# Gram products of a chunked delta rule spread over eight steps in half fills, and k, q loads moved behind the q products

## The reference

```
k_n = k / (norm(k) + 1e-6)
for t in range(768):
    y[t]  = q[t] @ state
    v_old = state^T k_n[t]
    state = state + beta[t] * outer(k_n[t], v[t] - v_old)
```

## Time and profile before

| | us |
|---|---|
| median of 3 runs | 1146.16 (1144.45 to 1147.41) |
| the profiled execution | 1137.16 |
| its span | 1135.4 |
| PE busy in the span | 1029.8 (91%) |
| DVE busy | 869.6 (77%) |
| ACT busy | 779.8 (69%) |
| POOL busy | 227.7 (20%) |
| first copy_low of the recurrence starts at | 60.27 |
| last copy_low of the recurrence starts at | 293.76 |

### The profile page before, as it was taken

How to read it: one execution, slowest core, us unless ns; L and a number is a source line. 1 busy time by engine, 2 the same in 40 slices (tenths; PEclk the granted TensorE clock), 3 DMA queues, 4 the chain that set the end, 5 groups by cost and what they waited for, 6 DMA issues and landing times.

```text
span 1135.4 us, 24237 instructions
## 1 busy us (share of the span) xinstructions
PE 1029.8 (91%) x10274; PEld 819.1 (72%) x10280; DVE 869.6 (77%) x948; ACT 779.8 (69%) x991; POOL 227.7 (20%) x380
## 2 busy tenths in 40 slices
PE   4478788898778999999999998899999999999997
PEld 2366566666657788777787776778888888888886
DVE  4965646565389888788887877999787878888885
ACT  1143524465488998999998897987676767676764
POOL 5088887780010001001001000000000000000000
PEclk7588979899889999999999999999999999999999
DMA  7823434232343343524324353530100101010000
GB/s 176 238 59 103 114 99 128 73 88 98 101 91 77 74 112 63 123 55 112 74 55 111 74 147 89 136 111 1 56 1 10 45 0 56 0 56 1 29 1 28
DMA packets 35104, 86.99 MB, mean 77 GB/s; under 512 B 4416, under 2 KB 12096, under 8 KB 35008
## 3 DMA queue, kind: packets, MB, share of 16 engines
q1 hardware_dynamic: 27584, 59.13, 17.3%
q0 software_dynamic: 6912, 25.17, 11.6%
q10 hardware_dynamic: 512, 1.31, 0.5%
HBM read 46.27 MB, written 14.16 MB: 53 GB/s over the span
## 4 chain that ended last, share of the span: by engine, by line
PE 33%; DVE 20%; ACT 12%; issue 6%; DMA 1%; ACTq 0%; DVEq 0%; POOLq 0%
PE o_ps L854 6%; PE o_ps L856 6%; PE o_ps L855 6%; PE h_ps L854 5%; PE h_ps L856 5%; PE h_ps L855 5%; DVE val L1078 5%; DVE den L1035 5%; ACT rec L942 4%; DVE pa L1041 4%; ACT rec L950 3%; DVE val L1062 2%; ACT pa L918 2%; DMA val<-pa 1%; DVE den L1069 1%
## 5 line engine op out<-in xcount | busy, mean ns | idle before, releaser
L854 PE MATMUL o_ps<-g_hi,w_hi_early 128*128 128x512 f32 x288 | 115.5, 401 | 21.8 <-DVE g_lo L1084 15.7
L931 ACT ACTIVATE g_hi<-val 128x1024 fp32r<-128x1024 f32 x96 | 101.9, 1062 | 42.5 <-DVE val L1078 36.8
L845 POOL DMA_DIRECT2D val<-pa x48 | 41.5, 864 | 427.4 <-DVE pa L1041 427.4
L854 PE MATMUL o_ps<-g_hi,w_hi_late 128*128 128x512 f32 x288 | 114.4, 397 | 8.8 <-DVE g_lo L1084 8.3
L1062 DVE TENSOR_TENSOR val<-val,rec 128x1024 f32<-128x1024 f32 x96 | 117.0, 1219 | 5.6 <-DMA val<-pa 5.6
L1078 DVE SCALAR_TENSOR_TENSOR val<-den,val 128x1024 f32<-128x1024 f32 x96 | 117.4, 1223 | 5.0
L1084 DVE SCALAR_TENSOR_TENSOR g_lo<-val,g_hi 128x1024 fp32r<-128x1024 f32 x96 | 117.7, 1226 | 2.0 <-ACT g_hi L931 2.0
L855 PE MATMUL o_ps<-g_lo,w_hi_early 128*128 128x512 f32 x288 | 113.5, 394 | 0.0
L856 PE MATMUL o_ps<-g_hi,w_lo_early 128*128 128x512 f32 x288 | 113.3, 393 | 0.0
L855 PE MATMUL o_ps<-g_lo,w_hi_late 128*128 128x512 f32 x288 | 112.9, 392 | 0.0
L856 PE MATMUL o_ps<-g_hi,w_lo_late 128*128 128x512 f32 x288 | 112.8, 392 | 0.0
(11 more groups left out here) (114 smaller groups left out, 2179.7 us busy)
## 6 DMA issues: line engine op xcount, KB each, us to landing
val<-pa POOLq DMA_DIRECT2D x48, 512.0 KB, 4.6
w_raw<-w SPq DMA_DIRECT2D x16, 768.0 KB, 5.1
kv_run<-kv_n SPq DMA_DIRECT2D x24, 384.0 KB, 3.7
x_raw<-x_dram SPq DMA_DIRECT2D x12, 768.0 KB, 5.7
kq<-kq_t SPq DMA_DIRECT2D x44, 192.0 KB, 4.7
x_dram<-stage SPq DMA_DIRECT2D x12, 384.0 KB, 4.3
x_dram<-stage SPq DMA_DIRECT2D x6, 768.0 KB, 4.1
out<-stage SPq DMA_DIRECT2D x5, 768.0 KB, 4.1
```

The source lines that it names most:

```text
L854: nc.tensor.matmul(dst, hi, rhs_hi, start=first, stop=False)
L931: act_fn(g_hi[:, n % 2], val[:, n % 2], ACT.Copy, scale=-1.0).then_inc(g_hi_ready, 1)
```

## The change

The fills are cut in two halves by chunk (`c2` 0 or 1), and the halves are spread by written lists. In tiles 2 and 3 (and by the same rule wherever the tile exists) steps 0 to 3 do the second half of tile tau+2 and steps 4 to 7 the first half of tile tau+3, half a fill a step. Tiles 0 and 1 have lists of their own, with some whole fills, in which the order reaches the new shift. `scale_gram` follows the second half of a fill. `weights` of tile tau+3 moves to step 5 (step 7 in tile 0), and the transpositions of tile 2's n_mat to step 7 of tile 0. The wait ahead of `keep_warm` names the fills that are in flight then. On SP the kq loads go ahead of the kv load and wait for the q product of the chunk (`q_done`) instead of its update.

```diff
+GRAM_0 = ((), ((2, 0, 0), (2, 0, 1)), ((2, 1, 0),), ((2, 1, 1),), ((2, 2, 0), (2, 2, 1)), ((2, 3, 0),), ((2, 3, 1),),
+          ((3, 0, 0), (3, 0, 1)))
+GRAM_1 = (((3, 1, 0), (3, 1, 1)), ((3, 2, 0),), ((3, 2, 1),), ((3, 3, 0), (3, 3, 1)),
+          ((4, 0, 0),), ((4, 0, 1),), ((4, 1, 0),), ((4, 1, 1),))
+GRAM = ((2, 2, 0), (2, 2, 1), (2, 3, 0), (2, 3, 1), (3, 0, 0), (3, 0, 1), (3, 1, 0), (3, 1, 1))
...
+def gram_parts(tau, s):
+    if tau < 2:
+        return (GRAM_0, GRAM_1)[tau][s]
+    ahead, f, c2 = GRAM[s]
+    return ((tau + ahead, f, c2),) if tau + ahead < T else ()
...
                 for c in range(CT):
+                    if tau + RING < T:
+                        sp.wait_ge(q_done, index(tau, c, 1) + 1)
+                        for r in range(HALVES):
+                            load_kq(sp, tau + RING, c, r)
                     if tau + 1 < T:
                         sp.wait_ge(st_done, index(tau, c, 1) + 1)
                         load_kv(tau + 1, c)
-                    if tau + RING < T:
-                        for r in range(HALVES):
-                            load_kq(sp, tau + RING, c, r)
...
-            def gram_fill(j, f):
+            def gram_fill(j, f, chunks=range(2)):
                 cp, r = f // 2, f % 2
                 if r == 0:
-                    for c2 in range(2):
+                    for c2 in chunks:
                         pe.wait_ge(kq_loaded[slot(j, 2 * cp + c2)], 32 * (j // RING) + 32)
-                if j >= 2:
+                if j >= 2 and 0 in chunks:
                     pe.wait_ge(gram_used, 4 * j + f)
...
-                for c2 in range(2):
+                for c2 in chunks:
...
-                last.then_inc(gram_done, 1)
+                if 1 in chunks:
+                    last.then_inc(gram_done, 1)
...
                     if tau and s == 0:
                         pe.wait_ge(inv_ready, tau)
-                        if tau + 1 < T:
-                            pe.wait_ge(gram_used, 4 * (tau + 1) + 4)
+                        pe.wait_ge(gram_used, 4 * 3 + 1 if tau == 1 else min(4 * (tau + 2) + 2, 4 * T))
                         by_event()
                         keep_warm(BURST)
                     solve(tau, c, g)
-                    if tau + 2 < T and 0 <= fill < 4:
-                        gram_fill(tau + 2, fill)
+                    for j, f, c2 in gram_parts(tau, s):
+                        gram_fill(j, f, (c2,))
...
-                    if fill == 0 and tau + 2 < T:
-                        weights(tau + 2)
-                    if tau + 2 < T and 0 <= fill < 4:
-                        scale_gram(tau + 2, fill)
+                    if (tau, s) == (0, 1):
+                        weights(2)
+                    if (tau, s) == (0, 7):
+                        turn_n(2, 0, half_k)
+                        turn_n(2, half_k, C)
+                    if s == (7 if tau == 0 else 5) and tau + 3 < T:
+                        weights(tau + 3)
+                    for j, f, c2 in gram_parts(tau, s):
+                        if c2 == 1:
+                            scale_gram(j, f)
...
-                    if fill == 3 and tau + 2 < T:
+                    if tau and s == 3 and tau + 2 < T:
                         turn_n(tau + 2, 0, half_k)
-                    if fill == 4 and tau + 2 < T:
+                    if tau and s == 4 and tau + 2 < T:
                         turn_n(tau + 2, half_k, C)
```

More of the change, by code:

```diff
@@ L464, in _ @@
                     q = index(tau, c, g)
-                    fill = s - (1 if tau == 0 else 0)
                     if tau and s == 0:
                         pe.wait_ge(inv_ready, tau)
-                        if tau + 1 < T:
-                            pe.wait_ge(gram_used, 4 * (tau + 1) + 4)
+                        pe.wait_ge(gram_used, 4 * 3 + 1 if tau == 1 else min(4 * (tau + 2) + 2, 4 * T))
                         by_event()
```

## The result

The changed kernel is faster: median 1131.72 us over 6 runs (1131.49 to 1137.32) beside 1145.31 for the kernel before in the same job (6 runs, 1141.35 to 1147.41). The ratio is 0.9914, 95% interval 0.9891 to 0.9938, some 10 us. (The medians alone lie 13.6 us apart, because four of the changed kernel's six runs are near 1131.6 and the other two at 1135.0 and 1137.3.) I had forecast 4 us slower.

What follows compares the result with a forecast made beforehand. The recurrence was taken as bound by TensorE's own in-order stream. Terms 1.03 + 3.1 + 1.1 + 0.0 − 2.06 + 0.9 = +4.1 us, added to the timed median 1146.16, gave 1150.2 us; range 1142 to 1155.5.

Steps and rivals of the forecast that it cites:

- the one on the loads: kq issued about 2 us earlier, ahead of kv, in time for its use: cost 0, bad end 1 us in each of tiles 1 and 2.
- Rival A: Faster: parted load bursts shrink instruction-fetch stalls (−5.2 us) and clock falls (−2.2): 1142.8 us; chance 0.22.
- The sign that I had set for being wrong: One of three: the recurrence's "issue" idle, 20.8 us over three listed products, falling under 18 us.
- C: Slower still: idle in step 2 of tiles 1 and 2 and the border trip the low clock: 1155 us; chance 0.13.
- Bound by PE's in-order stream: Recurrence: steps run back to back on PE, about 0.3 us of cover each; a half fill costs 0.52 us, nearly all exposed.
- Tile 0, step 7: 4.1 us of DVE transpositions, weights and scaling before the state copy, against 0.90 idle: about 3.1 us on the path.
- Step 2 of tiles 1 and 2: Losing a half fill gains nothing; PE's idle time for u_blk grows from 1.75 to 2.27 us.
- Tile 3: Four half fills fewer and no squares to wait for: −2.06 us.
- Tiles 1 and 2: Half fills removed and added, less what is hidden: +1.1 us in tile 1, 0.0 in tile 2.
- The clock at the border of tiles 0 and 1: PE idles some 2.2 us before the warm-up, which may run at the low clock: 0 to 2.4 us, taken as 0.9.

Runs made afterwards that it cites:

- the loads alone: Kernel before with only the kq loads moved behind the q products, Gram fills left whole in steps 0 to 3: 0.9906 of before.
- before_shift128: Kernel before with 128 semaphore increments on PE's queue during its wait for the first inverse: 1.0046 of before.
- no_jam: Changed kernel, tile 0 keeping whole fills and transpositions in place, weights(3) in step 6, tile 3's first fill halved over steps 6 and 7: 0.9936 of before.

## Why the prediction was wrong

**The step that failed** is the one on the loads: "Cost 0, with 1 us in each of tiles 1 and 2 as the bad end." I asked only whether kq comes in time and what waits on SP. It does come in time. The term measured −0.73%, 8 us over three placements, from what the transfers do to an engine that never waits for them. With it the sum of +4.1 becomes −4, and the mean over placements is −4.3 us (0.9949 against 0.9987). The other 5 to 6 us of the measured 10 are the placement of this kernel, which no sum over a profile gives.

**The rival was there and I argued it away.** Rival A had the cause, the parted bursts and the fetches, and its 3.4 us under the kernel before is near the mean over placements, though not near the measured 10. Its mechanism was half right: it took most of its gain from less stall time in all (−5.2 us). The sum doesn't fall. It is 26.8 to 28.7 us in the six profiles of the kernel before and the loads alone, and 24 to 32 in all kernels but before_shift128; what changes with the loads is the length of single pieces and the time at the low clock. The sign that I had set for being wrong, stall time under 18 us, was met by the three lines that I had listed (14.3) and not by the whole (28.1): I had left out the k product and the Gram fills. A piece of 2.14 us was followed by 6.8 us at the low level in the earlier trace rows; that price I gave to the rivals A and C and not to the forecast, which left the 24 us at the low clock in tiles 1 and 2 as they were.

The Trainium skill (DMA: Bandwidth & Descriptors, "Queues, rings and completion order") has the DMA engines take turns between queue rows. I concluded that a fetch wouldn't stand behind a burst and let that weigh against A. The fetch packets agree with the page as far as they go: they take 1.1 us with and without load data beside them. My conclusion doesn't hold: 384 KB more per chunk cost 0.6% with nothing waiting for it, and fetches beside load data were followed by a long piece ten times as often.

**Bound by PE's in-order stream**: right. A half fill in a clean step pushes the q product back by 0.58 us, more than the 0.52 I took (half of the 1.03 in the earlier trace rows):

```profile
163.38 0.65 PE L374 MATMUL side_ps<-kq 48*32 48x64 f32 x32
163.96 0.54 PE L418 MATMUL y_bank<-state,kq 128*32 128x96 f32 x16
```

Spreading products gained nothing, as forecast: the half fills cost 0.36% on average, 4.1 us. That it is my sum to the decimal is luck, since the mean is only good to some 3 us and the sum's parts were off both ways.

**Tile 0, step 7**: right for the stretch itself. The residual to the state copy takes 3.96 us, where "4 us" stood, with the transpositions, the weights and the scaling between them; compare 0.90 of idle time in the earlier trace rows.

```profile
97.33 0.35 DVE L678 TENSOR_TENSOR z<-kv_run,ks_ps 128x192 f32<-128x192 f32 x1 [2.44 <-PE ks_ps L392]
97.61 1.99 DVE L659 STREAM_TRANSPOSE n_turned<-n_mat 128x512 f32<-128x512 f32 x2
99.53 0.13 DVE L618 TENSOR_SCALAR norm<-scratch 128x32 f32<-128x32 f32 x1
...
100.96 0.41 DVE L642 TENSOR_TENSOR p_mat<-side_ps,upper 128x256 f32<-128x256 f32 x1
101.29 0.54 DVE L695 COPY state<-st_bank 48x384 f32<-48x384 f32 x1
101.76 0.27 DVE L650 TENSOR_TENSOR w_blk<-wgt,blk_mask 128x128 f32<-128x128 f32 x1
101.95 2.12 DVE L668 STREAM_TRANSPOSE x_mat<-inv 128x512 f32<-128x512 f32 x2
```

The warm-up behind it was the one whose price I put at 0.9 between 0 and 2.4. PE stood 1.12 us, until scale_gram was done at 101.37, and the 12 products took 4.08 us, not 2.54; the first solve of tile 1 starts 8.2 us after the residual (I had "7.5 or more"), 1.4 us after x_mat could have released it.

```profile
101.48 4.08 PE L357 MATMUL side_ps<-idle 128*128 128x512 bf16 x12 [1.12 <-issue]
105.49 0.54 PE L405 MATMUL hz_ps<-z,x_mat 32*32 32x48 f32 x32
```

In the six profiles with tile 0's new order it takes 46.4 to 50.3 us, mean 48.0, from u_blk to u_blk; in the six profiles of the kernel before and the loads alone 40.9 to 45.1, mean 42.6. That is +5.4 for a forecast of 5.0. That it counts in full in the total is not shown (no_jam).

**Step 2 of tiles 1 and 2**: not as sized. PE's wait for u_blk was to grow to 2.27 us. In tile 2 it is 1.39, behind an unexplained piece of 0.65 in the same step that took its place in part; in tile 1 a piece of 1.94 took it whole. DVE's wait for the squares (2.59 in both tiles) is nearly the 2.90 of the earlier trace rows.

```profile
161.17 0.87 PE L432 MATMUL st_bank<-u_blk,kv_run 128*64 128x192 f32 x8 [1.39 <-DVE u_blk L689]
```

**Tile 3**: −2.8 us over three placements beside the loads alone (36.4 against 39.2), forecast −2.1. Tiles 1 and 2 beside the loads alone: +1.3 and +0.8, forecast 1.1 and 0.0.

**The clock at the border of tiles 0 and 1.** I booked its fall to the idle time ahead of the warm-up. But the low level had begun at 97.4, three microseconds before that idle time, behind a fetch piece in the fill of the last step:

```profile
95.35 1.05 PE L374 MATMUL side_ps<-kq 48*32 48x64 f32 x58 [1.24 <-issue]
```

So the 1.5 us that the warm-up took longer are near my 0.9, for another reason, and by chance. I had named the Trainium skill (TensorE: Matmul & The Clock Gate, "HAM oscillation — how this bites in real kernels") for the full 2.4; that section tells of bursts that start cold behind waits for data longer than this gap, and its case isn't this one. What the traces do show is that the clock fell behind pieces in the middle of the work, and that is where the change gained: before, 10 pieces of 1.5 us or more and 52.0 us at the low level, after, 6 and 40.5.

**Range**: its lower end, 1142, lay just under rival A's 1142.8, so half of a rival with a chance of 0.22 was outside it, and A's own scatter I never priced. A spread of 0.5% from placement belonged in it.

## What to carry to other kernels

A transfer that nobody waits for still can have a price where an engine runs long straight-line code: look at how dense the load traffic is where the instruction packets stand, and at the idle pieces that nothing explains, by their length and by what the granted clock does behind each, not by their sum. Try to part loads that go out together when the data allow it, on either side: here one side gave 0.8% and the other 0.3%. And before crediting half a per cent to a schedule, shift the busiest engine's instructions by a few dozen and measure again.

## What was not expected of the hardware

PE stood 19.44 us over 128 semaphore increments in a row, so one takes up to 152 ns and is no free marker on that engine. With no work changed, 64 of them under cover moved the kernel by −0.49%, and not through the clock. Nearly every unexplained PE piece of 1.5 us or more (145 of 146) has an instruction packet under it. And with the same products on PE, the profile of the kernel before with 32 increments had 58.0 us at the low clock, that of the loads-only kernel 21.0: the clock, which I had treated as noise, is most of what the loads' move gains.
